# The bonus r·u·k moved into the diagonal of the block scores, and outputs copied by ScalarE

## The chip, the cores and the metric

The kernel runs on one core of a Trainium2 chip. The metric is the device time of one execution in microseconds (us); the median of several executions is compared. TensorE (PE), VectorE (DVE), ScalarE (ACT) and GpSimd (POOL) compute, SyncE (SP) only issues transfers here. Each engine takes its instructions in program order; semaphores order them between engines.

## What is computed

Attention with a decaying state, then an MLP, then a soft mixture of experts, all in fp32:

```python
for t in range(S):                       # B, H, S, D = 4, 8, 768, 48
    cur = u * k_t  (outer)  v_t          # the bonus, for step t alone
    y[:, :, t] = r_t @ (state + cur)
    state = w_t * state + k_t (outer) v_t
x = y as (3072, 384)
h = x @ w_in ; g = h * sigmoid(1.702 h) ; x2 = g @ w_out          # d_ff = 2048
logits = x2 @ phi ; softmax over tokens -> 32 slots -> 8 experts -> softmax over slots
```

The bonus part of y is, for one head, sum_d(r[d] u[d] k[d]) times v: one number for each step and head, times v.

## The kernel before

The sequence is worked in 24 chunks of 128 steps (four batches of six). In a chunk the eight heads lie as four pairs p, two heads (par 0 and 1) on partitions 0 to 47 and 64 to 111. Each chunk is split in two blocks of 64 steps (c).

The MLP sets the order of the work. It runs in nine token steps of two or three chunks (SIZES), each of 16 slots F (one per 128 of d_ff). In slot F, TensorE does nine matmuls for the hidden layer F (`hidden_layer`, L1417: high and low parts in fp32r) and nine (six where the step has two chunks) for the output of slot F-2 (L1552). ScalarE does gelu (L854) and its high part (L865), VectorE the low part (L1185). Everything else is put by hand into slots: `part_at` and `meeting_at` (L351 to L379) say in which slot each part of a chunk's attention is done, the loops over `slots_of_work` on ScalarE, VectorE and TensorE look it up, each behind its MLP work of that slot.

For chunk n: raw (w, r, k, v by feature) is loaded, one field at a time from chunk 4 on (`load_field`, L797, issued by ScalarE). VectorE makes the running decay (L987) and its inverse (L1012), rp = r x decay (L1021), kd = k / decay (L1028). TensorE turns kd (four transposes into the bank mps, L1451), ScalarE copies it out as kn (L811). At a *meeting* (`meet`, L1334) TensorE does the block scores of chunk n, the state sums of n and the outputs of chunk o = n-1 (from its masked scores and from the state). VectorE then adds the outputs to ybuf (`add_output`, L1082), sums the state (L1056 to L1080) and masks the scores of n (`mask_scores`, L1030: multiplied by a strictly triangular mask). SP stores ybuf to memory and loads it again as x for the MLP.

The bonus goes its own way: VectorE makes ruk = r x u x k (L996, four instructions; in chunks 0 to 3 only r x k, L1003), ScalarE its high part rukh (L904), VectorE the low part rukl (L1212). TensorE sums over the features of each head and spreads the sum over the head's rows (L1570 and L1572, 512 columns each, into mps; chunks 0 to 3: four fp32 matmuls with u in the stationary side, L1458). VectorE multiplies by v into ybuf (`bonus_values`, L1045), and `add_output` adds the rest to it.

Chunks 0 and 1 are done in `start_up` of each engine, ahead of the MLP, while the weights and the decays (for a check of their size) are loaded. There the queue of SP and the chains between the engines are written out by hand.

## Time and profile before

| | us |
|---|---|
| median of 3 runs | 597.05 |
| lowest, highest | 596.88, 599.43 |
| the profiled execution | 598.29 |
| its span, first to last instruction | 596.6 |
| TensorE busy in it | 573.4 (96%) |
| VectorE busy | 329.6 (55%) |
| ScalarE busy | 264.0 (44%) |
| mean granted TensorE clock | 0.992 of full |

The difference between a busy time and the span is idle time; where an engine never idles in a stretch, that engine's instructions set its length. Matmuls are pipelined, so their shown durations overlap and the distance between two starts is what one costs. In every row below, L and a number is the line of the kernel, and "<-" after the arrow names what the engine waited for.

### The profile page before, as it was taken

Reading aid. Unit: us, or ns where it says so; the run is one execution under the profiler, and the core shown is the slowest. Engines: PE = TensorE matmul, PEld = TensorE weight load, DVE = VectorE, ACT = ScalarE, POOL = GpSimd, SP = SyncE. Lnnn points to the kernel's source line nnn. Section 1 sums busy time; section 2 is a strip of 40 time slices with the busy share of each in tenths; the row PEclk is TensorE's granted clock in tenths of the full one; section 3 lists DMA queues with packets and bytes.
Section 4 is the critical chain, followed back from the end, with each engine's and each line's share of the span. In section 5 each row is a group of like instructions: output and inputs, shape, how many; then the busy total and the mean of one; then the engine's idle time right before and its main releaser. Section 6 shows DMA issues by size and latency. Waiting matters only on the chain.

```text
span 596.6 us, 15329 instructions
## 1 busy us (share of the span) xinstructions
PE 573.4 (96%) x6335; PEld 523.4 (88%) x6335; DVE 329.6 (55%) x713; ACT 264.0 (44%) x540; POOL 10.5 (2%) x28
## 2 busy tenths in 40 slices
PE   8889999999999999999999999999999999999983
PEld 6788989889989998999999999999999999998332
DVE  8778777657846664566445645576364224323304
ACT  3955444363463335333544344333533356554313
POOL 4010000000000000000000000000000000000000
PEclk9999999999999999999999999999999999999996
DMA  8994523323432322222212322232111197768728
GB/s 282 381 221 161 150 79 102 90 79 89 110 97 73 87 70 63 63 66 84 87 50 87 88 57 78 73 88 73 56 48 27 40 387 243 230 223 280 245 77 317
DMA packets 52983, 77.52 MB, mean 130 GB/s; under 512 B 4256, under 2 KB 33440, under 8 KB 52576
## 3 DMA queue, kind: packets, MB, share of 16 engines
q1 hardware_dynamic: 41872, 54.88, 28.8%
q10 hardware_dynamic: 10240, 18.50, 10.1%
q0 software_dynamic: 800, 3.15, 1.7%
q8 instruction: 51, 0.84, 0.6%
q14 instruction: 20, 0.16, 0.1%
HBM read 67.46 MB, written 9.04 MB: 128 GB/s over the span
## 4 chain that ended last, share of the span: by engine, by line
PE 83%; DMA 7%; DVE 3%; issue 3%; ACT 2%; SPq 2%; ACTq 0%; DVEq 0%
PE hps L1417 33%; PE acc L1552 32%; DMA spare<-w_in 4%; DMA w2s<-w 2%; PE zps L1340 2%; PE mps L1358 2%; PE yps L1352 1%; PE mps L1451 1%; PE mps L1635 1%; PE zps L1352 1%; PE mps L1668 1%; PE zps L1346 1%; DMA out<-obuf 1%; PE mps L1648 1%; PE hps L1712 1%
## 5 line engine op out<-in xcount | busy, mean ns | idle before, releaser
L1185 DVE TENSOR_TENSOR gl<-g,gh 128x384 fp32r<-128x384 f32 (+1 forms) x144 | 73.9, 513 | 209.0 <-ACT gh L865 208.9
L1417 PE MATMUL hps<-xh,wi_hi 128*128 128x384 f32 (+1 forms) x432 | 146.8, 340 | 3.5 <-ACT g L854 2.2
L1417 PE MATMUL hps<-xh,wi_lo 128*128 128x384 f32 (+1 forms) x432 | 137.2, 318 | 0.0
L1417 PE MATMUL hps<-xl,wi_hi 128*128 128x384 f32 (+1 forms) x432 | 137.0, 317 | 0.0
L854 ACT ACTIVATE g<-hps 128x384 f32<-128x384 f32 (+1 forms) x144 | 65.6, 455 | 146.4 <-PE hps L1417 146.2
L1552 PE MATMUL acc<-wo_hi,gl 128*128 128x384 f32 x384 | 129.2, 337 | 0.0
L1552 PE MATMUL acc<-wo_lo,gh 128*128 128x384 f32 x384 | 129.2, 336 | 0.0
L1552 PE MATMUL acc<-wo_hi,gh 128*128 128x384 f32 x384 | 129.0, 336 | 0.2 <-issue 0.2
L865 ACT ACTIVATE gh<-g 128x384 fp32r<-128x384 f32 (+1 forms) x144 | 70.5, 489 | 118.1 <-PE acc L1552 117.5
L1417 PEld LDWEIGHTS hps<-xh,wi_hi 128*128 128x128 f32 x432 | 81.2, 188 | 13.7 <-issue 5.3
L1417 PEld LDWEIGHTS hps<-xl,wi_hi 128*128 128x128 f32 x432 | 81.5, 189 | 0.9
L1417 PEld LDWEIGHTS hps<-xh,wi_lo 128*128 128x128 f32 x432 | 81.2, 188 | 0.0
L1552 PEld LDWEIGHTS acc<-wo_lo,gh 128*128 128x128 f32 x384 | 72.2, 188 | 0.3 <-issue 0.3
L1552 PEld LDWEIGHTS acc<-wo_hi,gh 128*128 128x128 f32 x384 | 72.2, 188 | 0.1
L1552 PEld LDWEIGHTS acc<-wo_hi,gl 128*128 128x128 f32 x384 | 72.1, 188 | 0.0
L1012 DVE TENSOR_TENSOR_SCAN inv<-raw,ends 112x516 f32<-112x516 f32 x24 | 29.6, 1233 | 0.8
L987 DVE TENSOR_TENSOR_SCAN decay<-raw,restart 112x516 f32<-112x516 f32 x24 | 29.4, 1224 | 0.6 <-DMA raw<-dmaj 0.6
L1358 PE MATMUL mps<-vn,kn 64*48 64x48 f32 x640 | 23.7, 205 | 1.1 <-issue 0.9
L996 DVE SCALAR_TENSOR_TENSOR ruk<-raw,ucols 112x128 f32<-112x128 f32 x80 | 23.2, 345 | 0.0
L1358 PEld LDWEIGHTS mps<-vn,kn 64*48 64x48 f32 x640 | 20.3, 121 | 1.4 <-issue 1.0
L1352 PE MATMUL zps<-rp,state 48*48 48x64 f32 x320 | 21.5, 216 | 0.0
L1352 PE MATMUL yps<-rp,midway 48*48 48x64 f32 x320 | 20.7, 216 | 0.0
(251 smaller groups left out, 734.2 us busy)
## 6 DMA issues: line engine op xcount, KB each, us to landing
w1s<-w SPq DMA_DIRECT2D x16, 768.0 KB, 6.6
w2s<-w SPq DMA_DIRECT2D x16, 768.0 KB, 6.2
raw<-dmaj ACTq DMA_DIRECT2D x40, 225.8 KB, 2.6
vn<-vnat SPq DMA_DIRECT2D x24, 192.0 KB, 2.5
tests<-wall SPq DMA_DIRECT2D x6, 768.0 KB, 15.0
out<-obuf SPq DMA_DIRECT2D x12, 384.0 KB, 4.0
raw<-dmaj ACTq DMA_DIRECT2D x20, 226.2 KB, 2.5
raw<-dmaj ACTq DMA_DIRECT2D x20, 225.3 KB, 2.5
```

Source lines behind the costliest of these rows:

```text
L854: act.activation(g32[F % 2][:, 0:wide], hps[F % 2][:, 0:wide], ACT.Gelu_apprx_sigmoid).then_inc(gelu_done, 1)
L865: act.activation(gh[F % 2][:, 0:wide], g32[F % 2][:, 0:wide], ACT.Copy).then_inc(gh_done, 1)
L987: dve.tensor_tensor_scan(flat[0], flat[1], flat[2], 1.0, ALU.mult, ALU.max).then_inc(scanned, 1)
L996: last = dve.scalar_tensor_tensor(ruk[n % 2][:, p, :], field(n, RR)[:, p], ucols[:, p:p + 1], field(n, KK)[:, p], ALU.mult, ALU.mult)
L1012: dve.tensor_tensor_scan(flat[0][:, ::-1], later, flat[1][:, ::-1], 1.0, ALU.mult, ALU.add).then_inc(inverted, 1)
L1185: dve.tensor_tensor(out=gl[F % 2][:, 0:wide], in0=g32[F % 2][:, 0:wide], in1=gh[F % 2][:, 0:wide].bitcast(fp32), op=ALU.subtract).then_inc ...
L1340: return pe.matmul(score_banks(n)[par][cols, p * HALF:(p + 1) * HALF], kd[n % 2][rows, p, cols], rp[n % 2][rows, p, cols], start=p == 0, s ...
L1346: return pe.matmul((zps, yps)[c][HALF * par:HALF * par + D, p * HALF:(p + 1) * HALF], vn[o % 2][rows, h * D:(h + 1) * D], scores[rows, par ...
L1352: return pe.matmul((zps, yps)[c][rows, p * HALF:(p + 1) * HALF], (state[o % 2], midway)[c][rows, p, :], rp[o % 2][rows, p, HALF * c:HALF * ...
L1358: return pe.matmul(sum_banks(n)[c][HALF * par:HALF * par + D, p * D:(p + 1) * D], kn[n % 2][rows, p, HALF * par:HALF * par + D], vn[n % 2] ...
L1417: last = pe.matmul(hps[F % 2][:, 0:wide], w[:, g, at:at + 128], v[i % 2][:, g, 0:wide], start=m == 0, stop=m == 3 * G - 1)
L1552: last = pe.matmul(acc[m][:, 0:DM], a[k][:, rows], w[:, f % CW, :], start=f == 0 and w is hi and a is gh, stop=f == NF - 1 and a is gl)
```

## The change

The bonus of step t is put on the diagonal of the scores of its block, where the strict mask has zeros: scores[t, t] = sum_d(r u k), so the product with v that the scores go through anyway adds it. For this the sum is wanted with the step on the partitions. Four fp32 matmuls behind the four transposes give it: stationary ruk (now r x k in all chunks), moving heads_u (two columns a pair, u of head 0 and of head 1), output 128 x 2 into mps behind the turned keys. ScalarE copies both out together (456 columns for 448). VectorE writes eye x bonus over the whole scores tile (128 x 512), then copies the scores where the mask is set over it (`copy_predicated`). The outputs have nothing to be added to, so ScalarE copies them from PSUM to ybuf (`take_output`, in the meeting's slot, behind its wait for the meeting); for chunks 0 and 1 VectorE does. Gone are rukh, rukl, the two wide matmuls, bonus_values, and v by feature with its load. The places of the parts in the slots are written anew.

```diff
-W, RR, KK, VV = range(4)
+W, RR, KK = range(3)
...
-        kn = [sb(f"kn{i}", [C, HP, R]) for i in range(2)]
+        turned = [sb(f"turned{i}", [C, HP * R + H]) for i in range(2)]
+        kn = [t[:, 0:HP * R].rearrange("t (p d) -> t p d", p=HP) for t in turned]
+        bonus = [t[:, HP * R:HP * R + H].rearrange("t (p r) -> t r p", r=2) for t in turned]
...
-        place_parts(2, scan=1, invert=1, grow=2, decayed=3, bonus_a=4, turn=4, bonus=6)
-        place_parts(3, scan=5, invert=7, grow=7, turn=8, decayed=8, bonus_a=8, bonus=10)
-        place_parts(4, scan=13, invert=14, grow=15, turn=16, decayed=15, bonus_a=11, bonus_b=13, split=16, bonus=17)
...
-        place_parts(PRE, mask=7)
...
+        place_parts(2, scan=1, invert=1, grow=2, products=2, decayed=3, turn=4, mask=8)
+        place_parts(3, scan=5, invert=6, grow=6, products=7, decayed=7, turn=8)
+        place_parts(4, load_w=7, load_k=9, load_r=10, scan=13, invert=14, grow=15, products=14, decayed=15, turn=16)
...
+            place_parts(n, load_w=f - 8, load_k=f - 7, load_r=f - 6, scan=f - 6, invert=f - 5, grow=f - 5, products=f - 3,
+                        decayed=f - 1, turn=f)
...
-        low_at = {0: 2, 4: 3, 6: 4, 9: 5, 10: 6, 12: 7}
+        low_at = {0: 2, 4: 3, 9: 5, 10: 6, 12: 7}
+        low_behind = {5: 4}
...
-                    sp.wait_ge(uv_done, n + 1)
+                    sp.wait_ge(decayed_done, n + 1)
+                    sp.wait_ge(front, n + 1)
+                    sp.wait_ge(ruk_made, n + 1)
...
-                act.activation(kn[n % 2][:, :, :], mps[:, 0:HP * R].rearrange("t (p d) -> t p d", p=HP),
-                               ACT.Copy).then_inc(kn_done, 1)
+                act.activation(turned[n % 2][:, :], mps[:, 0:HP * R + H], ACT.Copy).then_inc(kn_done, 1)
+
+            def take_output(n):
+
+                act.wait_ge(meetings, met_out[n])
+                if n >= 2 * PRE:
+                    act.wait_ge(y_stored[n % 2], 32 * (n // 2 - 1))
+                else:
+                    act.wait_ge(permuted, PRE)
+                for c in range(2):
+                    cols = slice(HALF * c, HALF * (c + 1))
+                    last = act.activation(ybuf[n % 2][:, :, cols], (zps, yps)[c][0:R, 0:HP * HALF].rearrange("e (p t) -> e p t", p=HP),
+                                          ACT.Copy)
+                last.then_inc(y_done, 1)
...
-                if (F, "split") in part_at:
-                    n = part_at[F, "split"]
-                    act.wait_ge(ruk_made, n + 1)
-                    act.wait_ge(u_done, n)
-                    act.activation(rukh[:, :, :], ruk[n % 2][:, :, :], ACT.Copy).then_inc(rukh_done, 1)
                 if (F, "turn") in part_at:
                     turned_keys(part_at[F, "turn"])
+                if F in meeting_at and meeting_at[F][0] is not None:
+                    take_output(meeting_at[F][0])
...
             def mask_scores(n):
 
+                dve.wait_ge(kn_done, n + 1)
+                if n and n <= PRE:
+                    dve.wait_ge(av_done, n)
+                elif n:
+                    dve.wait_ge(meetings, met_out[n - 1])
+                dve.tensor_tensor(out=scores[:, :, :, :], in0=eye[:, :].unsqueeze(1).unsqueeze(1).broadcast_to([C, 2, HP, HALF]),
+                                  in1=bonus[n % 2].unsqueeze(3).broadcast_to([C, 2, HP, HALF]), op=ALU.mult).then_inc(diagonal, 1)
                 if n < PRE:
                     dve.wait_ge(z_done, n + 1)
                 else:
                     dve.wait_ge(meetings, met_in[n])
-                if n and n <= PRE:
-                    dve.wait_ge(av_done, n)
-                elif n:
-                    dve.wait_ge(meetings, met_out[n - 1])
+                    dve.wait_ge(y_done, n)
+                dve.wait_ge(diagonal, n + 1)
                 for par in range(2):
-                    dve.tensor_tensor(out=scores[:, par], in0=score_banks(n)[par].rearrange("s (p t) -> s p t", p=HP),
-                                      in1=mask[:, :].unsqueeze(1).broadcast_to([C, HP, HALF]),
-                                      op=ALU.mult).then_inc(scored, 1)
+                    dve.copy_predicated(scores[:, par], mask[:, :].bitcast(i32).unsqueeze(1).broadcast_to([C, HP, HALF]),
+                                        score_banks(n)[par].rearrange("s (p t) -> s p t", p=HP)).then_inc(scored, 1)
...
                 for p in range(HP):
-                    last = pe.transpose(mps[:, p * R:(p + 1) * R], kd[n % 2][:, p, :], ident[0:R, 0:R])
-                last.then_inc(kd_turned, 1)
...
+                    pe.transpose(mps[:, p * R:(p + 1) * R], kd[n % 2][:, p, :], ident[0:R, 0:R])
                 pe.wait_ge(ruk_made, n + 1)
                 for p in range(HP):
-                    last = pe.matmul(bonus_bank(n)[0:R, p * C:(p + 1) * C], heads_u[p][:, :], ruk[n % 2][:, p, :],
-                                     start=True, stop=True)
-                last.then_inc(u_done, 1)
+                    at = HP * R + 2 * p
+                    last = pe.matmul(mps[:, at:at + 2], ruk[n % 2][:, p, :], heads_u[:, p, :], start=True, stop=True)
+                last.then_inc(kd_turned, 1)
```

## Rows read from the trace of the kernel before

**Rows 1.** The page, part 1: busy us (share of the span) and instructions of each engine.

```profile
PE 573.4 (96%) x6335; PEld 523.4 (88%) x6335; DVE 329.6 (55%) x713; ACT 264.0 (44%) x540; POOL 10.5 (2%) x28
```

**Rows 2.** Windows by stage; columns in the first line.

```profile
core 0: us, PE busy (x) PEld busy (x) DVE busy (x) ACT busy (x) POOL busy (x), PEclk, DMA share, GB/s
0.00:34.60 34.60, 27.95 (x396) 23.76 (x396) 26.27 (x59) 22.20 (x28) 7.31 (x24) 1.00 0.97 314
34.60:87.00 52.40, 49.79 (x620) 47.08 (x620) 42.05 (x72) 24.92 (x50) 3.17 (x4) 1.00 0.52 150
87.00:171.00 84.00, 82.56 (x1125) 75.99 (x1123) 58.80 (x142) 39.52 (x94) 0.00 (x0) 1.00 0.33 95
171.00:234.50 63.50, 63.50 (x700) 60.47 (x699) 36.73 (x81) 25.89 (x53) 0.00 (x0) 1.00 0.26 76
```

**Rows 3.** TensorE's groups: busy us, mean ns, idle us before and what ended it.

```profile
L1417 PE MATMUL hps<-xh,wi_hi 128*128 128x384 f32 (+1 forms) x432 | 146.8, 340 | 3.5 <-ACT g L854 2.2 <-DVE xl L544 1.0 <-DVE wi_lo L1157 0.4
...
L1340 PE MATMUL zps<-rp,kd 48*64 48x64 f32 x352 | 15.1, 224 | 0.5 <-DVE rp L1021 0.5
...
L1451 PE MATMUL mps<-ident,kd 112*128 112x112 f32 x96 | 13.3, 260 | 0.5 <-DVE kd L1028 0.5
```

**Rows 4.** Timeline of TensorE, a bonus slot: start, us, instruction.

```profile
243.26 0.39 PE L1570 MATMUL mps<-rukh,headsum 112*112 112x512 f32 x1
...
243.72 0.34 PE L1417 MATMUL hps<-xh,wi_hi 128*128 128x384 f32 x1
243.91 0.34 PE L1417 MATMUL hps<-xl,wi_hi 128*128 128x384 f32 x1
```

**Rows 5.** Timeline of TensorE, the bonus of chunk 2.

```profile
47.52 1.04 PE L1458 MATMUL mps<-ruk,heads_u 112*112 112x128 f32 x8
48.31 0.36 PE L1417 MATMUL hps<-xh,wi_hi 128*128 128x256 f32 x1
48.52 0.28 PE L1417 MATMUL hps<-xl,wi_hi 128*128 128x256 f32 x1
```

**Rows 6.** Timeline of TensorE at the end: small fp32 matmuls with 128-column weights.

```profile
550.82 0.85 PE L1619 MATMUL mps<-merge,gathered 96*128 96x32 f32 x6
551.50 0.36 PE L1623 MATMUL yps<-den,merge 96*128 96x1 f32 x2
551.73 0.91 PE L1401 MATMUL hps<-ident 128*128 128x128 f32 x6
```

**Rows 7.** VectorE's groups, each form apart.

```profile
L996 DVE SCALAR_TENSOR_TENSOR ruk<-raw,ucols 112x128 f32<-112x128 f32 x80 | 23.2, 345 | 0.0
...
L1053 DVE TENSOR_TENSOR ybuf<-mps,raw 112x512 f32<-112x512 f32 x22 | 15.1, 685 | 0.0
L1212 DVE TENSOR_TENSOR rukl<-ruk,rukh 112x512 fp32r<-112x512 f32 x20 | 13.7, 687 | 1.4 <-ACT rukh L904 1.2
...
L1091 DVE TENSOR_TENSOR ybuf<-zps,ybuf 112x256 f32<-112x256 f32 x24 | 10.1, 421 | 8.2 <-PE mps L1358 6.3 <-PE yps L1317 2.0
...
L1041 DVE TENSOR_TENSOR scores<-yps,mask 128x256 f32<-128x256 f32 x22 | 9.1, 413 | 0.0
```

**Rows 8.** ScalarE's groups, each form apart.

```profile
L865 ACT ACTIVATE gh<-g 128x256 fp32r<-128x256 f32 x48 | 20.0, 418 | 25.9 <-PE acc L1552 25.5
...
L904 ACT ACTIVATE rukh<-ruk 112x512 fp32r<-112x512 f32 x20 | 12.7, 633 | 0.7 <-issue 0.3
```

**Rows 9.** Timeline behind a meeting: its last matmuls, and ScalarE's next gelu.

```profile
248.83 0.54 PE L1358 MATMUL mps<-vn,kn 64*48 64x48 f32 x16
...
251.19 0.49 ACT L854 ACTIVATE g<-hps 128x384 f32<-128x384 f32 x1 [3.53 <-PE hps L1417]
```

**Rows 10.** Timeline of ScalarE in the start, with its waits.

```profile
9.62 0.54 ACT L811 ACTIVATE kn<-mps 128x448 f32<-128x448 f32 x1 [1.26 <-PE mps L1451]
...
16.75 0.54 ACT L811 ACTIVATE kn<-mps 128x448 f32<-128x448 f32 x1 [0.36 <-PE mps L1451]
...
32.33 1.48 ACT L782 ACTIVATE wi_hi<-spare 128x1536 fp32r<-128x1536 f32 x1 [2.03 <-DMA spare<-w_in]
```

**Rows 11.** Timeline of TensorE: a matmul with one-column weights.

```profile
30.02 0.19 PE L1513 MATMUL acc<-outside,ones 128*1 128x4 f32 x2
```

More of the change, by code:

```diff
@@ L52 @@
 ON_ACT, ON_DVE = (0, 1, 2, 4), (3, 5)
+NQ = 3
 GEN_DMAS = 16 * 2 * (1 + HP)
@@ L99, in attention_mlp_soft_experts @@
         attn_at = place[0]
-        raw = [sb(f"raw{i}", [R, 4, HP, C + 1]) for i in range(2)]
+        raw = [sb(f"raw{i}", [R, NQ, HP, C + 1]) for i in range(2)]
         vn = [sb(f"vn{i}", [C, DM]) for i in range(2)]
@@ L819, in start_up @@
             def start_up():
-                act.wait_ge(headsum_made, 1)
+                act.wait_ge(heads_zeroed, 1)
                 act.wait_ge(u_in, 16)
-                for p in range(HP):
-                    last = act.activation(heads_u[p][:, :], headsum_f[:, :], ACT.Copy, scale=ucols[:, p:p + 1])
+                for par in range(2):
+                    rows = slice(HALF * par, (HALF, R)[par])
+                    last = act.activation(heads_u[rows, :, par:par + 1], ucols[rows].unsqueeze(2), ACT.Copy)
                 last.then_inc(heads_made, 1)
@@ L987, in decays, with products @@
                 dve.tensor_tensor_scan(flat[0], flat[1], flat[2], 1.0, ALU.mult, ALU.max).then_inc(scanned, 1)
-            def bonus(n, half):
-                if n == FULL and half == 0:
-                    dve.wait_ge(u_in, 16)
+            def products(n):
                 await_field(n, RR)
                 await_field(n, KK)
-                for p in (2 * half, 2 * half + 1):
-                    last = dve.scalar_tensor_tensor(ruk[n % 2][:, p, :], field(n, RR)[:, p], ucols[:, p:p + 1], field(n, KK)[:, p],
-                                                    ALU.mult, ALU.mult)
-                if half:
-                    last.then_inc(ruk_made, 1)
-            def products(n):
                 dve.tensor_tensor(out=ruk[n % 2][:, :, :], in0=field(n, RR), in1=field(n, KK), op=ALU.mult).then_inc(ruk_made, 1)
@@ L1114, in start_up @@
                     dve.tensor_copy(fold[rows], ident[rows, rows])
+                for c in range(2):
+                    rows = slice(HALF * c, HALF * (c + 1))
+                    last = dve.tensor_copy(eye[rows], ident[rows, rows])
+                last.then_inc(eye_made, 1)
+                decays(1)
+                dve.wait_ge(eye_made, 1)
                 mask_scores(0)
-                decays(1)
                 first_state(0)
@@ L1199, in _ @@
                     decayed(part_at[F, "decayed"])
-                if (F, "bonus_a") in part_at:
-                    n = part_at[F, "bonus_a"]
-                    if n < FULL:
-                        products(n)
-                    else:
-                        bonus(n, 0)
-                if (F, "bonus_b") in part_at:
-                    bonus(part_at[F, "bonus_b"], 1)
-                if (F, "split") in part_at:
-                    n = part_at[F, "split"]
-                    dve.wait_ge(rukh_done, n - FULL + 1)
-                    dve.wait_ge(u_done, n)
-                    dve.tensor_tensor(out=rukl[:, :, :], in0=ruk[n % 2][:, :, :], in1=rukh[:, :, :].bitcast(fp32),
-                                      op=ALU.subtract).then_inc(rukl_done, 1)
+                if (F, "products") in part_at:
+                    products(part_at[F, "products"])
                 if F in low_at:
@@ L1217, in _ @@
                     before, n = meeting_at[F]
-                    if before is not None:
-                        add_output(before)
                     if n is not None:
@@ L1562, in _ @@
                     mps_read = (kn_done, n + 1)
-                if (F, "bonus") in part_at:
-                    n = part_at[F, "bonus"]
-                    pe.wait_ge(*mps_read)
-                    if n < FULL:
-                        bonus_sums(n)
-                    else:
-                        pe.wait_ge(rukl_done, n - FULL + 1)
-                        pe.matmul(mps[0:R, :], headsum[:, :], rukh[:, :, :].rearrange("d p t -> d (p t)"),
-                                  start=True, stop=False)
-                        pe.matmul(mps[0:R, :], headsum[:, :], rukl[:, :, :].rearrange("d p t -> d (p t)"),
-                                  start=False, stop=True).then_inc(u_done, 1)
-                    mps_read = (uv_done, n + 1)
                 if F in meeting_at:
```

95 lines of the change are left out of this document (29 added, 66 removed).

## The prediction, made before the changed kernel was run

> **What bounds the kernel now.** I read the page first, then the windows by stage, then the waits of TensorE, and last its instructions in order of time. The page gives TensorE 96% of the span, VectorE 55%, ScalarE 44% [rows 1]. A share alone proves little, so the windows: in the full step from 171 to 234.5 us TensorE is busy without a gap (63.50 us of 63.5), at the full granted clock (2.4 GHz), while VectorE has 36.7 us and ScalarE 25.9 us of work in the same time [rows 2]; the later steps repeat it up to about 540 us. Before 87 us there are gaps (49.79 of 52.40 us), between 87 and 171 us few (82.56 of 84). The waits of TensorE that concern us all lie in the first 80 us: 2.2 us for ScalarE's first gelu, 1.0 us for the low part of x, 0.5, 0.5 and 0.4 us for VectorE (rp, kd, a weight part) [rows 3]. So two regimes: an early stretch in which VectorE, ScalarE and the loads decide, and about 450 us in which each instruction that TensorE issues costs its distance to the next one and nothing else counts. Busy time is a poor measure there, because matmuls overlap: a 128x384 one is shown 0.34 us long and the next starts 0.17 us later. I therefore take start-to-start distances throughout.
>
> **The change part by part. Removed from TensorE.** Chunks 4 to 23, 20 of them, lose the pair L1570/L1572. It starts at 243.26, the next layer at 243.72: 0.46 us, and the matmul behind it is 0.19 instead of 0.17 us apart, so 0.47 us [rows 4]. 20 x 0.47 = 9.4 us. Chunks 0 to 3 lose four fp32 matmuls each (L1458), which the trace shows as eight records: an fp32 matmul runs as two, each with its own weight load. In chunk 2 they take 47.52 to 48.31 plus a stretched first distance (0.21 for about 0.12) = 0.88 us [rows 5].
>
> **Added to TensorE.** Every chunk gets four small fp32 matmuls behind the turned keys. The operands matter: ruk[:, p, :] (112x128) is now the stationary side and heads_u (two columns) the moving one. So eight weight loads of 128 columns each, with hardly anything moving. No row has this shape; the nearest ones are at the end of the kernel: L1619 (96x128 weights, 32 moving columns, six records) and L1623 (96x128 weights, one moving column, two records). They start at 550.82 and the next instruction starts at 551.73: eight records in 0.91 us, 0.114 us each. L1623 alone: 551.50 to 551.73, 0.115 us each with a single moving column [rows 6]. That is the same pace as L1619's 32 columns, so what is paid is the weight load. I take 0.91 us per chunk. Lower bound: the records of L1458, 0.79/8 = 0.099 us [rows 5], which makes 0.79 us. Upper bound: 0.115 x 8 plus one stretched first distance of 0.09 us behind the group = 1.01 us.
> This is where the page of the Trainium skill "TensorE: Matmul & The Clock Gate" speaks against the change: its section "LDWEIGHTS (loading the stationary operand)" gives a load as columns / 1.2 ns, 107 ns for 128, whatever the rows; the trace agrees (0.114 us), and eight loads would be an estimated 0.85 us by it.
>
> Net per chunk of the saturated stretch 0.91 - 0.47 = +0.44 us, 20 times: **+8.8 us** (bounds 0.32 and 0.54: +6.4 to +10.8). Chunks 2 and 3: 0.91 - 0.88 each, +0.1 us together. The four transposes that the group stands behind are unchanged.
>
> **VectorE.** Per chunk from 4 on it loses four products with u (L996, 4 x 0.345), the low part (L1212, 0.687), the bonus times v (L1053, 0.685), the two additions (L1091, 0.42 each) and the two masked copies (L1041, 0.41 each) [rows 7]: 1.38+0.69+0.69+0.84+0.82 = 4.4 us. It gains one full product (0.68, the form of L1053 [rows 7]), the diagonal (128x512, two broadcast inputs: 0.68 to 0.7 by the same form) and two predicated copies of 128x256 out of PSUM. Those no row shows: 0.41 us each if they go as L1041, 0.82 if at half its rate; I take 0.41. So 2.2 us (3.0 at worst), 1.4 to 2.2 us less than before. In the saturated stretch VectorE has 26.8 us free per step [rows 2], so this brings nothing and would cost nothing even at the upper bound.
>
> **ScalarE.** It loses rukh (0.633 [rows 8]), its turned copy grows by 8 columns on 448 (0.01 us), and it gains two copies of 112x256 out of PSUM, about 0.4 us each (as the 128x256 copy of L865, 0.418 [rows 8]): +0.2 us a chunk. The order is what could bite: take_output waits for the meeting, and behind it in ScalarE's queue stand that slot's work on x and the next gelu. The cover: after a meeting the next gelu can't begin before the nine matmuls of the next layer anyway. ScalarE is shown idle for 3.53 us before the gelu at 251.19, and the meeting's last matmuls start at 248.83 and end at about 249.4, 1.8 us before that gelu [rows 9]. The two copies (0.8 us) fit in with about 1 us over. In the one slot (F=26) where a split of x stands behind them (0.52 us) and the layer is only 256 wide (1.05 us), gelu comes up to 0.4 us late; the buffer that it fills is needed a slot later. Without this cover it would be 0.8 us for each of 22 chunks. VectorE now waits for y_done before the predicated copies; the state sums (0.7 us) and the diagonal (0.68 us) go first, longer than ScalarE's 0.8 us plus a handover. Nothing in the saturated stretch.
>
> **DMA and SP.** A quarter of each chunk's features isn't loaded: 4 x 226 KB become 3, one DMA issue less in ScalarE's queue. The queues are under a third busy there [rows 2]: no effect. At the start they are full, below. SP's reload of raw is no longer held by uv_done but by three earlier signals.
>
> **The early stretch.** Two chains meet at ScalarE's third weight part (L782). One is the load, spare<-w_in, landing at 32.3 us, for which ScalarE idles 2.03 us [rows 10]; 0.45 MB less are queued ahead of it, at the 314 GB/s of this stretch [rows 2] about 1.4 us earlier. The other is attention chunks 0 and 1. There mask_scores(0) now waits for the turned copy, which waits for the small matmuls: they end 0.9 us behind the transposes, so the copy (9.62 before [rows 10]) ends at about 11.0, diagonal and predicated copies at 12.4, and the first state sum, at 11.76 before, comes some 0.65 us late. The second turned copy, at 16.75 before [rows 10], sees that and its own 0.9 us: about +1.6 us. From that copy to the second weight part ScalarE works in one piece, so it reaches the third one at 30.3 + 1.6 = 31.9 instead of idling until 32.33: -0.4 us for the first gelu. Then VectorE's load falls while chunks 2 and 3 are prepared: with the low weight part of slot 6 moved ahead, kd and rp of chunk 3 a slot earlier and two bonus steps gone, the waits for wi_lo, kd and rp should go: they hold TensorE for 0.54, 0.63 and 0.6 us by start distances (the waits shown, 0.4, 0.5 and 0.5 [rows 3], plus what the pipelined ends hide). What is late next there is x: its low part (wait of 1.0 us [rows 3]) now has the whole product of chunk 4 ahead of it in slot 14, 0.68 us, where half of it stood in slot 13: +0.3 us. Together -0.4 - 1.8 + 0.3 = **-1.9 us**, bounds -3.5 (all waits of rows 3 but that for x go) and +1.5 (the start's chain is the later one in full).
>
> **Sum.** +8.8 + 0.1 - 1.9 = +7.0 us. The profiled execution took 598.29 us (span 596.6 and 1.7 around it), so 605.3 for it; it lies 1.2 above the median of 597.05, and for that median I forecast **604.0 us**.
>
> **Rivals.** (A) The small matmuls are paced by what moves, two columns. For it: L1513, two records with four moving columns, are 0.02 us apart [rows 11]; against: its weights are one column wide, and L1623 with one moving column isn't faster than L1619 with 32. Price: 8 x 0.025 = 0.2 us a chunk, 20 x (0.2 - 0.47) + 2 x (0.2 - 0.88) = -6.8 us, with the early -1.9: -8.7, **588.4 us**. It decides as soon as eight records take less than 0.47 us. The skill's same page, section "Back-to-back issue gap", has about 25 ns as the floor for 1 to 64 columns, which would make this rival true were the load not paid; no run here shows it for 128-column weights. Chance 0.08.
> (B) ScalarE's new wait or the longer start chain reaches TensorE: take_output late by 0.2 us in half of the 20 slots (+2) and the start at its upper bound (+3.4 on my value): +12.4, **609.5 us**. Against it is the 3.53 us idle. 0.09.
> (C) The early stretch gives its lower bound and the small group runs at L1458's pace: +6.4 + 0.1 - 3.5 = +3.0, **600 us**, on the edge of no change. 0.06.
> (D) The forecast, 0.77.
>
> **From these to the numbers.** 0.5% (3 us) is about what a measurement of this kernel tells from no change. Faster: A, 0.08. Same: half of C and a little of D's lower edge, 0.07. Slower: the rest, 0.85. Range: D's bounds for the group with a middling start give 601 to 606.5; taking in C and most of the way to B gives 600 to 608.
>
> **What the profile after would show.** Right: 192 PE records with 128-column weights behind the transposes (four calls, two records, 24 chunks), eight in 0.85 to 0.95 us from start to start; a full three-chunk step of 63.5 + 3 x 0.44 = 64.8 us; no new wait of TensorE after 90 us; VectorE's busy time down by some 40 us with nothing to show for it. Wrong if the step is at or under 63.5 us (then the loads are hidden, rival A), if TensorE waits for ScalarE's gelu or for scores in meeting slots (B), or if its first gelu moves by more than 2 us either way.

## The result, and the profile after

The changed kernel takes 609.5 us in the median, the kernel before 597.0 in the same rounds: ratio 1.0207, 95% interval 1.0157 to 1.0257. The forecast was 604.0 with a range from 600 to 608. Slower was right, the size was 5.5 us short, and the time lies above the range. The profiled execution took 607.74 us, span 606.0; before it was 598.29 and 596.6.

The page of the changed kernel, engines and two of its rows by slice:

```profile
PE 584.7 (96%) x6455; PEld 538.6 (89%) x6455; DVE 296.3 (49%) x588; ACT 268.5 (44%) x562; POOL 10.4 (2%) x28
...
PEclk9799999999999999999999999999999999999996
```

Against [rows 1], TensorE has 11.3 us more busy time, VectorE 33.3 us less, and the span is 9.4 us longer: nothing of VectorE's relief shows in the span. New is the 7 in the second slice of the granted clock, which was 9 before.

The windows by stage of the changed kernel, columns as in [rows 2]:

```profile
34.60:87.00 52.40, 49.14 (x608) 46.65 (x606) 38.49 (x61) 26.60 (x55) 3.17 (x4) 1.00 0.41 124
...
171.00:234.50 63.50, 63.25 (x711) 60.22 (x710) 30.70 (x60) 27.19 (x60) 0.00 (x0) 1.00 0.23 62
```

TensorE fills the last of these windows (63.25 of 63.50 us) as it did before. To size what TensorE does in it I take the start of the same transposes in later steps: before 192.56 and 319.52, after 197.13 and 326.72. Two full steps of three chunks take 126.96 and 129.59 us, so a step went from 63.5 to 64.8 us, +0.44 us a chunk. That is the forecast's figure.

The small group in the changed kernel, in order of time (start, duration), and its groups of the page:

```profile
278.61 0.55 PE L1415 MATMUL mps<-ident,kd 112*128 112x112 f32 x4
278.99 0.96 PE L1419 MATMUL mps<-heads_u,ruk 112*128 112x2 f32 x8
279.82 0.42 PE L1381 MATMUL hps<-xh,wi_hi 128*128 128x384 f32 x1
...
L1419 PEld LDWEIGHTS mps<-heads_u,ruk 112*128 112x128 f32 x192 | 23.3, 192 | 0.7 <-DVE ruk L993 0.7
L1419 PE MATMUL mps<-heads_u,ruk 112*128 112x2 f32 x192 | 23.3, 243 | 0.3 <-DVE ruk L993 0.2
```

Eight records take 0.83 us from start to start, 0.104 each, with the transposes ahead stretched by 0.07 us (0.38 to the group, where before it was 0.31 to the next layer), 0.90 together. The forecast took 0.91.

What the forecast did not see stands in the start. TensorE in stretches of 2 us (busy, instructions, granted clock, DMA share, GB/s), first the changed kernel, then the one before:

```profile
12.00:14.00 2.00, 0.80 (x30) 1.00 0.99 384
14.00:16.00 2.00, 1.29 (x46) 1.00 1.06 415
16.00:18.00 2.00, 1.91 (x44) 1.00 1.04 420
18.00:20.00 2.00, 1.24 (x34) 0.59 0.99 406
20.00:22.00 2.00, 1.76 (x13) 0.50 1.01 412
22.00:24.00 2.00, 2.00 (x14) 0.50 1.04 380
24.00:26.00 2.00, 2.00 (x65) 0.71 1.08 391
```

```profile
12.00:14.00 2.00, 1.43 (x65) 1.00 1.00 411
14.00:16.00 2.00, 1.21 (x42) 1.00 1.06 399
16.00:18.00 2.00, 1.94 (x33) 1.00 1.01 402
18.00:20.00 2.00, 1.52 (x40) 1.00 1.04 427
```

TensorE's clock falls to the lower of its two levels (1.2 of 2.4 GHz) for some 7 us in the profiled execution of the changed kernel, and not in that of the kernel before. TensorE's instructions of the start then take longer, and ScalarE's first gelu, at 33.72 before, comes at 36.14. What TensorE did ahead of the fall: from 12 to 14 us it was busy 0.80 of 2 us where it had been busy 1.43, and 1.24 against 1.52 from 18 to 20.

TensorE's waits up to 110 us in the changed kernel (in total, times, longest):

```profile
PE hps L1381 <- ACT g L861: 1.4, 1, 1.4
PE hps L1381 <- DVE xl L536: 1.3, 1, 1.3
PE yps L1275 <- DVE grown L1054: 1.2, 1, 1.2
...
PE yps L1275 <- DVE scores L1036: 0.3, 1, 0.3
...
PE mps L1419 <- DVE ruk L993: 0.2, 1, 0.2
```

The waits for wi_lo, rp and kd of [rows 3] are gone, the one for x has grown by 0.3, both as forecast; the last two rows are new (at 64.56 and 93.15 us). The third is the start's chain: the first state (`grown`) is formed later, since VectorE now makes it behind the predicated copies; TensorE's wait there was 0.57 us before.

### The profile page after: what moved, and what is told of

Its sections match the earlier page's. It is cut to its first block, busy times and chain, and to the rows that moved or that the text cites. A ratio compares the mean times of both kernels' runs of the same rounds, so it can differ in the third digit from the quotient of the medians.

```text
span 606.0 us, 15367 instructions
## 1 busy us (share of the span) xinstructions
PE 584.7 (96%) x6455; PEld 538.6 (89%) x6455; DVE 296.3 (49%) x588; ACT 268.5 (44%) x562; POOL 10.4 (2%) x28
## 4 chain that ended last, share of the span: by engine, by line
PE 87%; DVE 5%; issue 2%; ACT 1%; DMA 1%; POOL 1%; DVEq 0%; ACTq 0%; POOLq 0%
PE hps L1381 32%; PE acc L1510 31%; PE mps L1419 3%; PE zps L1304 2%; PE mps L1322 2%; PE mps L1415 1%; PE yps L1316 1%; PE acc L1627 1%; PE mps L1614 1%; PE mps L1581 1%; DMA out<-obuf 1%; PE zps L1316 1%; PE zps L1310 1%; PE mps L1594 1%; PE hps L1658 1%
## 5 line engine op out<-in xcount | busy, mean ns | idle before, releaser
L816 ACT ACTIVATE ybuf<-zps 112x256 f32<-112x256 f32 x22 | 8.5, 385 | 37.8 <-PE mps L1322 35.4
L1419 PEld LDWEIGHTS mps<-heads_u,ruk 112*128 112x128 f32 x192 | 23.3, 192 | 0.7 <-DVE ruk L993 0.7
L1419 PE MATMUL mps<-heads_u,ruk 112*128 112x2 f32 x192 | 23.3, 243 | 0.3 <-DVE ruk L993 0.2
L1322 PE MATMUL mps<-vn,turned 64*48 64x48 f32 x640 | 23.4, 205 | 0.1
L805 ACT ACTIVATE turned<-mps 128x456 f32<-128x456 f32 x24 | 13.3, 553 | 21.3 <-PE mps L1419 21.3
```

Of the source, the lines that this page charges most:

```text
L805: act.activation(turned[n % 2][:, :], mps[:, 0:HP * R + H], ACT.Copy).then_inc(kn_done, 1)
L1322: return pe.matmul(sum_banks(n)[c][HALF * par:HALF * par + D, p * D:(p + 1) * D], kn[n % 2][rows, p, HALF * par:HALF * par + D], vn[n % 2] ...
L1419: last = pe.matmul(mps[:, at:at + 2], ruk[n % 2][:, p, :], heads_u[:, p, :], start=True, stop=True)
```

## The experiments

Each heading says which kernel was changed. Times are medians, ratios are to the kernel before of the same rounds (597.3 to 597.4 us in these runs).

**The changed kernel again, as it is.**

> The changed kernel as it is, for comparison on the same chip. Theory (T1): the miss comes from the start-up, where TensorE idles so much while it waits for the longer chain of chunks 0 and 1 that its clock falls to 1.2 GHz for a time that differs between executions: the time spreads by 3 to 5 us between executions and the mean granted clock with it (0.979 to 0.986), about 609. Rival (T2): the price is in the saturated stretch or a constant one, the spread is chance: 607 to 609 with all runs within 1 us.

Measured: 609.6 us, ratio 1.0195 (1.0166 to 1.0223). In this trace the clock was already 0.80 at 12 to 14 us and 0.50 from 14 to 26, and the first gelu came at 38.27. So where the fall begins varies between the two traces. The other executions weren't profiled, but all ten of the changed kernel have a mean granted clock of 0.979 to 0.986, where the six with the fillers of the next run have 0.992 to 0.995.

**Fillers in the start of the changed kernel.** 24 matmuls on data that is never read, in TensorE's gaps:

```diff
                 state_sums(0)
-                keep_warm(WARM)
+                keep_warm(4 * WARM)
                 outputs(0)
-                keep_warm(WARM)
+                keep_warm(3 * WARM)
...
                 turn_keys(1)
+                keep_warm(2 * WARM)
                 pe.wait_ge(y_done, 1)
                 state_sums(1)
+                keep_warm(WARM)
```

> The changed kernel with 24 more filler matmuls (256 columns, into acc[0], operands zero) at the start: 9 behind the state sums of chunk 0, 6 behind its outputs, 6 behind the turned keys of chunk 1, 3 behind its state sums. T1: the clock stays at 2.4 GHz from 2 us on, the first gelu comes at about 34.5 to 35 us instead of 36.1, and the median falls from about 609 by 2 to 5 us, to 604.5 to 606.5, with a spread under 1 us. T2: no change or a bit slower (fillers cost up to 1 us), 608 to 610.

Measured: 605.6 us, ratio 1.0141 (1.0113 to 1.0169). The clock is 1.00 throughout the start, the first gelu at 33.86, the span 603.6 us. So 4.0 us of the 12.2 by which the changed kernel was slower in these rounds went with the clock. The other 8.2 us by medians (7.0 by the spans of the profiled executions) are the change at the full granted clock.

**Fillers in one gap only.** The same edit, once only the first two lines of it (behind chunk 0's sums and outputs), once only the last two (around chunk 1's).

> The changed kernel with 15 filler matmuls, 9 behind the state sums and 6 behind the outputs of chunk 0, and none of the other 9. Theory first gap: the fall starts with TensorE's wait for the predicated scores of chunk 0 (busy 0.80 of 2 us in 12 to 14 us, and 0.63 in the second trace, where the clock was 0.80 already in that stretch). With that gap filled the clock stays at 1.00 to 28 us and the time is that of the kernel with all 24 fillers, 605 to 606 us. Theory second gap: the clock still falls at 18 to 20 us and the time is near the changed kernel's, 608.5 to 609.5 us.

> The changed kernel with only the 9 filler matmuls behind the turned keys and the state sums of chunk 1. Theory first gap: the clock still falls (it fell to 0.80 in 12 to 14 us in one trace) and the time stays at 608.5 to 609.5 us, or above that since the fillers run at half the clock. Theory second gap: the clock stays at 1.00 and the time is 605 to 606 us.

Measured: 608.1 us (1.0169, 1.0145 to 1.0193) with the first gap filled, 607.1 (1.0170, 1.0143 to 1.0196) with the second. TensorE by 2 us, the first and then the second kernel:

```profile
12.00:14.00 2.00, 1.70 (x55) 1.00 1.05 398
...
18.00:20.00 2.00, 0.72 (x32) 0.70 1.04 427
20.00:22.00 2.00, 1.94 (x9) 0.50 0.98 398
```

```profile
12.00:14.00 2.00, 0.80 (x25) 0.94 0.99 389
14.00:16.00 2.00, 2.00 (x47) 0.50 1.08 419
16.00:18.00 2.00, 2.00 (x42) 0.71 1.01 408
18.00:20.00 2.00, 2.00 (x44) 1.00 1.03 424
```

Neither theory alone is right: in these two executions each unfilled gap has a fall of its own behind it. The fall in the second gap lasted longer and cost more (first gelu at 36.22, against 34.59 with the fall behind the first). The two medians, of six executions each whose spreads overlap (606.3 to 608.8 and 606.1 to 609.3), don't part the gaps. Each kernel also has one execution with a mean granted clock as high as with all the fillers (0.993 and 0.995), and these took 606.25 and 606.09 us: the fall behind an unfilled gap doesn't come every time.

**The small matmuls twice.** The changed kernel, from chunk 2 on:

```diff
-                for p in range(HP):
+                for p in (range(HP) if n < PRE else 2 * list(range(HP))):
                     at = HP * R + 2 * p
                     last = pe.matmul(mps[:, at:at + 2], ruk[n % 2][:, p, :], heads_u[:, p, :], start=True, stop=True)
```

> The changed kernel with the four small matmuls issued twice in chunks 2 to 23 (the same result written again). Theory L: 8 more records of 0.114 us in 22 chunks, +20 us. If the next instruction's weight load hides part of the first group and the second group does not get that, up to +22 us. Theory M (25 ns each): +4.4 us.

Measured: 630.2 us, ratio 1.0545 (1.0509 to 1.0581), 20.6 us over the changed kernel.

```profile
275.48 1.86 PE L1419 MATMUL mps<-heads_u,ruk 112*128 112x2 f32 x16
277.20 0.42 PE L1381 MATMUL hps<-xh,wi_hi 128*128 128x384 f32 x1
```

Sixteen records take 1.72 us where eight took 0.83: 0.89 us for the second eight, 22 x 0.89 = 19.6 of the 20.6. In this trace the clock also falls once more, at 60 to 66 us, which can be part of the rest. The group has its full price, and the price is not the 0.025 us a record that rival A took for its two moving columns.

**The small matmuls in two column halves.** The changed kernel, each one cut into two with 64 columns of weights:

```diff
+                    for c in range(2):
+                        cols = slice(HALF * c, HALF * (c + 1))
-                    last = pe.matmul(mps[:, at:at + 2], ruk[n % 2][:, p, :], heads_u[:, p, :], start=True, stop=True)
+                        last = pe.matmul(mps[cols, at:at + 2], ruk[n % 2][:, p, cols], heads_u[:, p, :], start=True, stop=True)
```

> The changed kernel, but each small fp32 matmul is cut in two of 64 weight columns each, which land in different column halves of the array (16 records of 64-column weights a chunk instead of 8 of 128). Theory L (the price is the weight load, by columns, and loads of different column tiles run side by side): 8 steps of about 0.055 us = 0.45 us instead of 0.91, 24 chunks: -10 to -11 us against the changed kernel. Theory L' (loads are paid one after the other): 16 x 0.055 = 0.88 us, no difference. Theory M (paid by moving columns or by instruction): 16 records at the old step of 0.11, +0.9 us a chunk, +20 us.

Measured: 605.7 us, ratio 1.0139 (1.0112 to 1.0166).

```profile
276.12 0.55 PE L1415 MATMUL mps<-ident,kd 112*128 112x112 f32 x4
276.60 0.63 PE L1421 MATMUL mps<-heads_u,ruk 112*64 112x2 f32 x16
277.16 0.44 PE L1381 MATMUL hps<-xh,wi_hi 128*128 128x384 f32 x1
```

The sixteen records take 0.56 us, 0.035 each, where half of 0.104 would be 0.052: the half loads do overlap. But the transposes ahead take 0.48 instead of 0.38, and from the first matmul behind the group to the second it is 0.28 instead of 0.26, so from the transposes to the second matmul of the layer it is 1.32 us instead of 1.47: -0.15 a chunk or -3.6 in 24, most of the 3.9 measured. The expectation had the group's gain right in direction and left out what the change from full to half width costs. The fall of the clock is in this kernel too (0.50 from 18 to 24 us).

**Both together, the fillers and the halves.**

> The changed kernel with both: the 24 filler matmuls of e1_warm and the small matmuls in column halves of e2_halves. If clock and group price are two independent terms, their gains (4.0 and 3.9 us against the changed kernel's 609.6) add up: 601.5 to 602, spread under 1.5 us. If the halves gained through the start (a shorter chain) rather than 0.17 us a chunk, 604 to 605.

Measured: 602.1 us, ratio 1.0079 (1.0052 to 1.0107). The two gains add up within 0.4 us (4.0 and 3.9 off 609.6 leave 601.7), so they are separate terms, and even with both the new pattern stays 0.8% over the kernel before.

**The removed pair issued twice.** The kernel before, L1570 and L1572 in a loop of two rounds:

```diff
+                        for again in range(2):
                             pe.matmul(mps[0:R, :], headsum[:, :], rukh[:, :, :].rearrange("d p t -> d (p t)"),
                                       start=True, stop=False)
```

> The kernel before, with the pair L1570/L1572 of the bonus issued twice for chunks 4 to 23 (the same sum written twice). The prediction took 0.47 us a chunk off TensorE for removing that pair. If this is the right price, one more pair costs 20 x (0.46 to 0.47) = +9.2 to +9.4 us: 606.2 to 606.6 where the kernel before gives 597. If part of the pair's time is really the exchange of weights at its edges, the second pair costs only its moving columns, about 4 x 0.09 to 0.11 us a chunk, under +9. If the pair lay in idle time, the added one would cost under +3.

Measured: 606.9 us, ratio 1.0151 (1.0114 to 1.0189), 9.6 us more; its span is 8.6 us longer.

```profile
264.01 0.39 PE L1571 MATMUL mps<-rukh,headsum 112*112 112x512 f32 x1
264.24 0.39 PE L1573 MATMUL mps<-rukl,headsum 112*112 112x512 f32 x1
264.47 0.39 PE L1571 MATMUL mps<-rukh,headsum 112*112 112x512 f32 x1
264.70 0.39 PE L1573 MATMUL mps<-rukl,headsum 112*112 112x512 f32 x1
264.93 0.34 PE L1417 MATMUL hps<-xh,wi_hi 128*128 128x384 f32 x1
```

0.23 us for each of the four: 0.46 us a pair, 9.2 us in 20 of the 9.6 measured. The pair was nowhere hidden, and its term in the sum stands.

**Outputs copied by VectorE.** The changed kernel with the fillers, `take_output` moved from ScalarE's queue to VectorE's:

```diff
-                if F in meeting_at and meeting_at[F][0] is not None:
-                    take_output(meeting_at[F][0])
...
                     before, n = meeting_at[F]
+                    if before is not None:
+                        later_output(before)
```

> e1_warm with the outputs of chunks 2 to 23 copied by VectorE at its place in the meeting slot instead of by ScalarE. If ScalarE's new wait for the meeting costs nothing (forecast): the same as e1_warm, 605.6, within 0.5 us. If it holds gelu back (rival B): 1 to 3 us less than e1_warm.

Measured: 606.8 us, ratio 1.0160 (1.0132 to 1.0188), 1.2 us more than with ScalarE's copies. On VectorE the copies stand ahead of the scores, and TensorE's wait for scores at L1287 grows from 0.3 to 1.0 us. That ScalarE's wait for the meeting costs nothing in the saturated stretch is read from the start of chunk 4's transposes to that of chunk 23's: 375.93 us with ScalarE's copies, 375.99 with VectorE's.

**The fillers out of the kernel before.** `keep_warm(WARM)` taken out behind bonus_sums(0), state_sums(0) and outputs(0).

> The kernel before without the nine filler matmuls behind the bonus sums, the state sums and the outputs of chunk 0. T1 (the idle time of TensorE in the start decides on its clock): the clock falls to 1.2 GHz somewhere between 12 and 26 us and the median rises by 2 to 5 us with a spread of 3 to 5 us, as the changed kernel shows. T2 (the clock drop belongs to something else in the changed kernel): 597, within 0.5 us.

Measured: 598.35 us, ratio 1.0014 (0.9995 to 1.0032), about 1 us. In the profiled execution (599.48 us) the clock falls here too (0.71 at 14 to 16 us, 0.50 from 16 to 20, 0.58 from 20 to 22), yet the first gelu comes at 34.13 instead of 33.72: before, ScalarE idled 2.03 us for its third weight part [rows 10], and the slower chain had that to use up. In the changed kernel that reserve is gone. This is the price at the gelu alone. Behind it TensorE stood for longer than before, where it had waited for the gelu until 34.64, and the profile names no engine:

```profile
36.81 0.38 PE L1417 MATMUL hps<-xh,wi_hi 128*128 128x256 f32 x1 [2.78 <-issue]
```

So chunk 2's transposes start at 43.20 instead of 41.14. Whether this pause has to do with the fall isn't shown. The median also mixes executions: the mean granted clock runs from 0.984 to 0.992 over the twelve, and the four at 0.987 or less took 599.1 to 601.9 us, the others 596.7 to 598.7. The expectation of 2 to 5 us was too high for the median, but not for those four.

**The new early slots in the kernel before.** Chunk 3's inverse and kd a slot earlier, the low weight part behind the meeting, as the change has them:

```diff
-        place_parts(3, scan=5, invert=7, grow=7, turn=8, decayed=8, bonus_a=8, bonus=10)
+        place_parts(3, scan=5, invert=6, grow=6, turn=8, decayed=7, bonus_a=8, bonus=10)
...
-        low_at = {0: 2, 4: 3, 6: 4, 9: 5, 10: 6, 12: 7}
+        low_at = {0: 2, 4: 3, 9: 5, 10: 6, 12: 7}
+        low_behind = {5: 4}
```

> The kernel before, only with the changed kernel's earlier places: chunk 3's inverse and kd in slot 6 and rp in slot 7, the low weight part 4 behind the meeting of slot 5 instead of in slot 6. Theory S (the waits of TensorE for wi_lo, kd and rp, 1.8 us together, are late VectorE work): they go, -1.0 to -1.8 us against 597. Rival (VectorE is full there, one wait takes the place of another): within 0.5 us of before.

Measured: 599.4 us, ratio 1.0041 (1.0021 to 1.0060): slower, where a gain was expected. TensorE's waits from 30 to 110 us, and ScalarE's queue (ACTq: issuing a transfer) in that kernel:

```profile
PE zps L1343 <- ACT kn L812: 2.8, 1, 2.8
...
50.07 3.59 ACTq L803 DMA_DIRECT2D raw<-dmaj  x1
53.70 1.49 ACT L783 ACTIVATE wo_hi<-stage 128x1536 fp32r<-128x1536 f32 x1 [3.55 <-issue]
...
55.98 0.54 ACT L812 ACTIVATE kn<-mps 128x448 f32<-128x448 f32 x1
```

The waits for wi_lo, rp and kd are gone as they should. But ScalarE's issue of chunk 4's field w, 0.32 us in its median of 80, lasts 3.59 us here, and behind it in ScalarE's queue stand a weight part, a gelu and the turned keys that TensorE then waits for. Before, the same issue took 2.25 us, of which the wait for the inverse is the larger part; in the changed kernel with fillers it took 0.38. What held it in this kernel isn't settled: the inverse that it waits for ended at 50.18. It isn't the whole price either. Right behind TensorE's wait of 2.8 us the clock falls (0.89, 0.50 and 0.75 from 56 to 62 us), and the twelve executions part in two: six with a mean granted clock of 0.989 to 0.994 took 598.2 to 598.9 us, six with 0.986 to 0.988 took 599.9 to 602.9.

**The split of x a slot earlier.** `{12: 0, 14: 1}` becomes `{12: 0, 13: 1}`, in the kernel before and in the changed one with fillers and halves.

> The kernel before, with one edit: the second part of the split of x for chunk 3's step (ScalarE's copy and VectorE's rest) stands in slot 13 instead of 14. The prediction held that TensorE's wait of 1.0 us for the low part of x comes from how late VectorE gets to it. If so, that wait goes and nothing else is in its place: 1.0 us less, 596 us. If something else is as late (the rows of the scratch that x is read from, or ScalarE's next gelu behind the moved copy), the time is that of the kernel before, within 0.3 us.

> The changed kernel with the 24 filler matmuls at the start and the small matmuls cut in two column halves (the two edits together gave 602.1 us), and the second part of the split of x in slot 13 instead of 14. In that kernel TensorE waits 1.3 us for the low part of x. If VectorE's order sets that wait, 600.8 us; if something else is as late, 602.1 us. By the terms found so far the pattern with the bonus on the diagonal then still stands about 4 us over the kernel before, which is what 20 groups cost TensorE more than 20 pairs.

Measured: 595.8 us (0.9977, 0.9959 to 0.9996) and 601.4 us (1.0067, 1.0042 to 1.0091). In both the wait for xl is gone from TensorE's waits; 1.5 and 0.7 us are gained. VectorE's order did set that wait. In the second kernel a new wait of 0.5 us, for chunk 4's kd, takes part of its place (1.3 us gone, 0.5 come); in the first, 0.5 us more is gained than the wait of 1.0 explains.

**Forty small writes on VectorE.**

```diff
+                if F is not None and 60 <= F < 68:
+                    for e in range(5 * (F - 60), 5 * (F - 59)):
+                        dve.memset(unused[:, e:e + 1], 0.0)
```

> The kernel before, with 40 writes of a single element on VectorE, five a slot in the slots 60 to 67, where it has time to spare. In the three traces with the instruction lists of the kernel before, the stretch from the last matmul to the end is 10.15 to 10.2 us and a packet of instructions is loaded in the last 16 us (queue 14); in the six traces with the changed lists there is none and the stretch is 9.3 to 9.45 us. Theory: that packet holds up the last store on its DMA engine; 40 more instructions of VectorE move the place at which it is loaded, so that there is none in the end stretch, which falls to about 9.4 us: 0.8 us less in the span, if the packet is VectorE's. Rival: the packet is another engine's or has nothing to do with the end; the stretch stays at 10.2 us and the time at that of the kernel before within 0.3 us (the 40 writes lie in time that VectorE has to spare).

Measured: 596.2 us, ratio 0.9981 (0.9964 to 0.9999). The last 16.6 us of the kernel before, and of this one (GB/s in 40 slices, then the queue of instruction packets where there is one):

```profile
GB/s 0 0 0 0 0 0 0 318 415 385 385 415 385 392 407 392 385 415 378 400 422 363 429 385 355 442 378 370 407 392 392 415 407 378 422 318 30 15 0 0
...
q14 instruction: 1, 0.01, 0.1%
```

```profile
GB/s 0 0 0 0 0 0 0 0 0 341 422 378 407 392 378 429 385 392 400 392 400 407 385 392 415 385 392 422 385 400 400 378 422 378 392 429 370 304 0 0
```

Before, two slices trickle at 30 and 15 GB/s behind the bulk: about what one of 16 DMA engines moves (an estimate: 400 GB/s of the bulk by 16 is 25). With the writes the packet has left this stretch, so have the two slices, and from the start of the last matmul to the end it is 9.4 us instead of 10.2. More work on VectorE made the kernel 0.8 us shorter at the end. Every trace here fits: in the five of kernels whose VectorE has the 713 instructions of the kernel before, the packet is there and the stretch is 10.1 to 10.2 us; in the other twelve it isn't, and the stretch is 9.3 to 9.5.

**The last two together, in the kernel before.**

> The kernel before with both edits that helped it: the second part of the split of x in slot 13 (595.8 us alone, 1.5 us under the kernel before in those rounds) and the 40 writes of one element on VectorE (596.2 us alone, 1.1 us under it). They work in different stretches (about 70 us, and behind the last matmul), so if both are real they add up: 2 to 2.5 us under the kernel before, 594.8 to 595.2 us where that gives 597.3. If one of the two was chance, 1 to 1.5 us under it.

Measured: 595.5 us, ratio 0.9968 (0.9953 to 0.9983): 1.8 us under the kernel before, where the two gains sum to 2.6, and below either alone by only 0.3 and 0.7. It is the fastest kernel here. That both gains are full and add is not shown by it. In its trace the clock falls at 34 to 38 us (0.55 and 0.60), behind TensorE's wait of 2.2 us for the first gelu: chunk 2's transposes start at 41.36, against 39.98 with the split of x alone, although its first gelu came earlier (32.16 against 32.43). So part of the 1.5 may have been the start's own spread.

## Why the prediction was right in sign and short in size

The kernel with fillers is the changed kernel at the full granted clock, which is what the prediction had in mind. Its trace against the one before, by the start of the same transposes:

| stretch | before | with fillers | difference | forecast |
|---|---|---|---|---|
| to chunk 2's transposes | 41.14 | 41.97 | +0.83 | -0.4 |
| to chunk 3's | 53.84 | 53.48 | -1.19 | -1.2 |
| to chunk 4's | 78.19 | 78.13 | +0.30 | -0.3 |
| to chunk 23's | 446.55 | 454.06 | +7.57 | +8.4 |
| to the last matmul | 586.41 | 594.22 | +0.30 | +0.4 |
| to the end | 596.6 | 603.6 | -0.8 | 0 |
| sum | | | +7.0 | +7.0 |

(The forecast's +8.8 is parted here as 19 chunks and one. Of its -1.8 for chunk 3's waits, wi_lo and kd lie ahead of chunk 3's transposes, at 51.01 and 53.84 us, and rp behind them, at 56.98. Its +0.1 for chunks 2 and 3 stands in the sum alone.) The equal sums are luck: the start cost 1.2 us more than forecast and the stretch to chunk 4's transposes 0.6 more, and 0.8 us in the steps and 0.8 us at the end came back that no term held. The early stretch, to chunk 4's transposes, was forecast at -1.9 us; it came to -0.1 with fillers and to +2.2 in the changed kernel as it is (80.38 us). This is the term that failed. The points are these.

**The removed pair and the small group: right.** 0.47 and 0.91 us were taken, 0.46 and 0.90 measured, net +0.44 a chunk in the steps. The nearest rows (L1619, L1623) gave the price of weights that are loaded for nothing to move, and doubling showed that it is paid in full. The Trainium skill, page "TensorE: Matmul & The Clock Gate", section "LDWEIGHTS (loading the stationary operand)", gives 107 ns for a load of 128 columns; the 0.104 us here agrees.

**The saturated stretch: 0.8 us less than forecast.** From chunk 6's to chunk 7's transposes it took 24.02 us before and 23.37 with fillers, where +0.44 was due. The kernel before has there an idle time of TensorE of 0.9 us that no other engine ends:

```profile
PE mps L1358 <- issue: 0.9, 1, 0.9
```

A pause of this kind, 0.5 to 0.9 us long, stands between chunk 3 and chunk 23 in five of the seven traces of the kernel before and those made from it (not in the one with early slots, nor in the one with the 40 writes), and in two of the ten of the changed kernel and those made from it, the two with one gap filled (0.8 and 0.6 us, at 61 to 63 us). So it isn't a thing that the change as such took away: it lay in the profiled execution of before, which the sum was made against, and the prediction hadn't listed it. What it is stays open.

**Chunk 3's waits: gone, but 0.6 us came in.** The three are gone, as forecast, and up to chunk 3's transposes the gain is the forecast one. In the stretch to chunk 4's, where -0.3 was due and +0.30 came, there is a new wait of 0.3 us for chunk 3's scores, of the kind that rival B had named; the other 0.3 isn't accounted for. "No new wait after 90 us" failed by a little: the wait of 0.2 us for ruk stands at chunk 5's group:

```profile
93.15 1.05 PE L1419 MATMUL mps<-heads_u,ruk 112*128 112x2 f32 x8 [0.24 <-DVE ruk L993]
```

**The start: the step that failed.** The forecast took two chains, the load and ScalarE's, and gave the first gelu -0.4 us; with fillers it was +0.14, and +0.83 at chunk 2's transposes. There is a third, TensorE's own: its first layer starts at 31.43 with fillers and at 30.14 before, and the first gelu now waits for it, even at the full clock:

```profile
33.86 0.39 ACT L861 ACTIVATE g<-hps 128x256 f32<-128x256 f32 x1 [0.85 <-PE hps L1381]
```

ScalarE is ready for it 0.85 us earlier. The load, which had set the first gelu before, is indeed earlier: in the changed kernel no wait for it is left. Where TensorE's chain became late shows one step earlier, at the placing of the outputs. It started at 19.02 before, without a wait; now it waits for chunk 1's predicated scores, which wait for the turned copy and so for the small group:

```profile
20.27 1.60 PE L1404 MATMUL hps<-ybuf,place_rows 112*128 112x128 f32 x12 [0.37 <-DVE scores L1036]
```

The prediction had this case in its bound of +1.5 us, "the start's chain is the later one in full", but that bound doesn't follow from its terms: the +1.6 us of that chain with -1.8 and +0.3 gives +0.1. The -0.1 measured with fillers is near that.

**The clock: what was left out.** The sum was made at the full granted clock because the trace of before shows 1.00 throughout the start. It did not ask what the longer waits behind the predicated copies would make of it. They stretch TensorE's idle time in 12 to 14 us from 0.57 us to 1.20 and in 18 to 20 from 0.48 to 0.76, and behind them the clock falls. With the gaps filled it doesn't, and this is worth 4.0 of the 5.5 us missed. The remaining 1.5 us is the early stretch again, seen by medians: they are 8.2 us apart with fillers, not the 7.0 of the two profiled executions, since that of the kernel before lay high. Its chunk 2 transposes, at 41.14, are later than in the three other traces with its start and no fall of the clock (39.98 to 40.90), while those of the kernels with fillers lie at 41.64 to 42.11. The forecast took 1.2 us off for a high profile, but had read its start from it.

**The rivals.** A fell with the doubled group. B named the measured number, 609.5, by luck: its ScalarE part (the wait for the meeting, +2) cost nothing, by the copies moved to VectorE, and its start part (+3.4 us) is where the loss was, but most of it through the clock, which B didn't name. Of the named marks, the step of 64.8 us and the 192 records came true, and their 0.83 us is a little under the 0.85 to 0.95 named; VectorE fell by 33.3 us, not 40; and the first gelu moved by 2.4 us, which the prediction had named as a sign of being wrong.

## What to carry to other kernels

Count a small matmul by the weights that it loads: with 128 fresh columns and two columns moving it costs 0.10 us a record, and an fp32 one is two records, so eight records with hardly anything moving cost 0.90 us a chunk. Turning the product round wouldn't have helped: the four fp32 matmuls of chunk 2 before, with 128 columns moving, cost 0.88. What was cheap, 0.46 us, was the pair of wide matmuls on high and low parts, 512 columns each. When a change lengthens a chain ahead of TensorE in a stretch where it already has gaps, ask for the granted clock as well as for the lateness, and find what reserve lies behind that stretch: in the profiled executions a fall of about 7 us moved the first gelu by 0.4 us where ScalarE had been waiting for a load, and by 2.3 us (36.14 against 33.86 with fillers) where it hadn't. And follow every chain that ends at the first full-size layer, the engine's own included, before taking the difference of two.

## What the runs showed of the hardware that was not expected

- Going from full-width weights to half-width ones has a price of its own: 0.10 us more from the transposes to the group, and 0.02 us more behind it, while each of the sixteen half-width records takes 0.035 us.
- The granted clock fell in either of two gaps at the start, for about 3 to 14 us, and where it fell first differed between two executions of one kernel (at 18 and at 12 us). In the profiled execution of the kernel before it doesn't fall; without nine of the fillers that this kernel has, it fell at 14 us.
- The kernel before isn't free of falls. Two kernels made from it, with its start unchanged, had one at 34 to 40 us in their traces, behind TensorE's wait of 2.0 to 2.2 us for the first gelu. Of its own 24 executions in the rounds with the split of x, seventeen with a mean granted clock of 0.991 or more have a median of 597.2 us and seven below that of 598.7; those seven weren't profiled.
- One packet of instructions loaded during the last stores makes the end 0.8 us longer, and where it is loaded moves with the length of an engine's list: that VectorE's list is the cause is shown by the 40 added writes; that the packet holds up a store on its DMA engine is argued from the two slow slices.
- An issue of a transfer by ScalarE, 0.32 us in the median, took 3.59 us in one kernel with nothing in the profile to hold it. It stays open.
- TensorE stood for 0.5 to 0.9 us in the steps of seven traces, and once for 2.8 us in the start, with no engine named that it waited for. It stays open too.
